# Attention with 49 agents and two split MLPs: inputs laid out transposed by the host, 25 chunks of 500 in place of 26 of 480

## The reference

```python
def sm(a, b):
    s = scale * (a @ b.transpose(0, 2, 1))
    s = s - s.max(-1, keepdims=True)
    e = np.exp(s)
    return e / (e.sum(-1, keepdims=True) + 1e-09)
agent_v = sm(agents, k) @ v            # 49 x 128, softmax over 12480 keys
x = sm(q, agents) @ agent_v            # 12480 x 128, softmax over 49 agents
h = x @ w_in                           # d_ff 2048
g = np.where(h >= 1, h, np.where(h <= -1, 0.0, (h + 1) ** 2 / 4.0))
x = g @ w_out
r = np.maximum(x @ w_in2, 0.0)
out = (s * (r * r) + b) @ w_out2
```

## Time and profile before

| what | value |
|---|---|
| median of 3 runs | 1188.39 us (1187.94 to 1191.43) |
| profiled execution, first to last instruction | 1189.1 us |
| PE busy | 1165.3 us, 98% |
| DVE, ACT, POOL busy | 954.6, 953.0, 841.0 us (80%, 80%, 71%) |
| start, to the first loop matmul (L573) | 106.6 us |
| DMA | 30.44 MB, nearly all of the reading in the first 100 us |

### The profile page before, as it was taken

The page is one execution under the profiler, slowest core; times in us unless marked ns, Lnnn a source line. Parts: engine busy times, 40 slices in busy tenths (PEclk is TensorE's granted clock), DMA queues, the critical chain, the costliest instruction groups (busy, mean ns, idle before and its releaser), DMA issues.

```text
span 1189.1 us, 20297 instructions
## 1 busy us (share of the span) xinstructions
PE 1165.3 (98%) x5668; PEld 1003.0 (84%) x5668; DVE 954.6 (80%) x1573; ACT 953.0 (80%) x1856; POOL 841.0 (71%) x1264
## 2 busy tenths in 40 slices
PE   9988899999999999999999999999999999999998
PEld 8986588888888888888888888888888888888886
DVE  2365888888888888888888888878888888888876
ACT  2225888888888888888888888888888888888886
POOL 2231088788778877887888788778877887887860
PEclk9999999999999999999999999999999999999999
DMA  7653000000000000000000000000000000000000
GB/s 187 193 141 95 1 1 18 1 17 18 17 0 17 17 17 0 17 17 1 17 17 17 1 17 17 17 1 17 17 0 17 17 17 0 18 9 9 1 9 17
DMA packets 12282, 30.44 MB, mean 26 GB/s; under 512 B 1529, under 2 KB 1578, under 8 KB 11962
## 3 DMA queue, kind: packets, MB, share of 16 engines
q1 hardware_dynamic: 12218, 29.78, 9.5%
HBM read 23.39 MB, written 6.39 MB: 25 GB/s over the span
## 4 chain that ended last, share of the span: by engine, by line
PE 87%; ACT 5%; issue 3%; DVE 3%; DMA 1%; ACTq 0%; SPq 0%; DVEq 0%
PE ps_h L592 7%; PE ps_h L593 7%; PE ps_h L594 7%; PE ps_o L634 7%; PE ps_y L554 7%; PE ps_o L635 7%; PE ps_o L636 7%; PE ps_y L556 7%; PE ps_h L573 7%; PE ps_y L555 7%; PE ps_h L574 7%; PE ps_h L455 2%; PE ps_h L443 2%; PE ps_job L455 2%; ACT sb_g_hi L732 1%
## 5 line engine op out<-in xcount | busy, mean ns | idle before, releaser
L1057 POOL TENSOR_TENSOR sb_g_lo<-sb_square,sb_g_hi 128x480 fp32r<-128x480 f32 x396 | 487.1, 1230 | 33.0
L917 DVE SCALAR_TENSOR_TENSOR ps_h<-sb_square,ps_h 128x480 f32<-128x480 f32 x416 | 274.6, 660 | 107.0 <-ACT sb_square L712 105.4
L732 ACT ACTIVATE sb_g_hi<-ps_h 128x480 fp32r<-128x480 f32 x416 | 238.4, 573 | 122.9 <-DVE ps_h L917 111.6
L900 DVE SCALAR_TENSOR_TENSOR sb_g_lo<-ps_h,sb_g_hi 128x480 fp32r<-128x480 f32 x416 | 273.0, 656 | 33.6 <-ACT sb_g_hi L732 24.0
L906 DVE TENSOR_SCALAR sb_below<-ps_h 128x480 f32<-128x480 f32 x400 | 262.0, 655 | 12.8 <-PE ps_h L574 10.2
L737 ACT ACTIVATE sb_relu<-ps_h 128x480 f32<-128x480 f32 x416 | 238.1, 572 | 21.4 <-PE ps_h L594 13.6
L712 ACT ACTIVATE sb_square<-sb_below 128x480 f32<-128x480 f32 x416 | 250.3, 602 | 0.9 <-DVE sb_below L906 0.4
L746 ACT ACTIVATE sb_square<-sb_relu 128x480 f32<-128x480 f32 x416 | 249.9, 601 | 0.6
L1055 POOL TENSOR_SCALAR sb_g_hi<-sb_square 128x480 fp32r<-128x480 f32 x396 | 232.4, 587 | 0.0
L1054 POOL TENSOR_TENSOR sb_gate<-sb_ones 1x1 f32<-1x1 f32 x396 | 73.8, 186 | 187.6 <-ACT sb_square L746 180.8
L554 PE MATMUL ps_y<-sb_g_hi,sb_w_out_hi 128*128 128x480 f32 x416 | 167.2, 402 | 2.4 <-DVE sb_g_lo L900 1.5
(11 more groups left out here) (114 smaller groups left out, 1484.6 us busy)
## 6 DMA issues: line engine op xcount, KB each, us to landing
sb_kv_ring<-in_k SPq DMA_DIRECT2D x13, 480.0 KB, 5.3
sb_q_ring<-in_q SPq DMA_DIRECT2D x26, 240.0 KB, 3.0
sb_kv_ring<-in_v SPq DMA_DIRECT2D x13, 480.0 KB, 5.6
out<-sb_out_ring SPq DMA_DIRECT2D x26, 240.0 KB, 2.4
sb_w_stage<-in_moe_w_in SPq DMA_DIRECT2D x1, 1024.0 KB, 7.2
sb_w_in<-in_moe_w_in SPq DMA_DIRECT2D x1, 1024.0 KB, 10.0
sb_w_stage<-in_moe_w_out SPq DMA_DIRECT2D x2, 0.5 KB, 11.6
sb_agents<-in_agents SPq DMA_DIRECT2D x1, 24.5 KB
```

The source lines that it names most:

```text
L732: nc.scalar.activation(g1_hi[:, place % SPLIT_RING], h1_ps[place % H1_BANKS][:, 0:W], ACT.Relu).then_inc(g1_hi_ready, 1)
L900: nc.vector.scalar_tensor_tensor(g1_lo[:, place % SPLIT_RING], h1_ps[place % H1_BANKS][:, 0:W], 0.0, as_f32(g1_hi[:, place % SPLIT_RING]), ...
L917: nc.vector.scalar_tensor_tensor(h, square1[:, place % WORK_RING], 1.0, h, ALU.min, ALU.add).then_inc(g1_summed, 1)
L1057: nc.gpsimd.tensor_tensor(g2_lo[:, place % SPLIT_RING], square, as_f32(hi), ALU.subtract).then_inc(g2_split, 1)
```

## The change

The host hands over `q` and `k` transposed (128 x tokens; `q` padded to 12500), `v` and the output weights already arranged by tile, `agents` transposed, `s` and `b` as two columns, and turns the output back itself. On the chip:

- `turn_k`, the copies to `k_t`, `turn_q`, the copy to `q_t`, the transposes of the output and their copy, and the transpose of the agents are gone.
- Keys come in 12 blocks of 8 tiles of 128 and one block of 2 tiles of 96; all of `k` has room at once, so nothing holds its loads back. The loads of `v` reuse the room of `k`.
- `weigh_v` has the values as the stationary operand (128 columns) and the exponentials moving (49 columns), and so gives `agent_v` transposed. The denominators come from `sum_exp`, one matmul with ones per block.
- A chunk is 500 tokens (4 sub-tiles of 126, overlapping), 25 chunks.
- The bias from `b` and `w_out2` comes from 16 small matmuls in iteration 0 (`sum_w_out2`) instead of a reduction on DVE; all parts of `m` are rounded by ACT and split by DVE, instead of ACT copies and POOL; `w_out1` is loaded and split in four parts; the guard of the query softmax is a 50th column.

```diff
-CHUNKS_PER_LOAD = 2
-KV_RING = 4
+W = 500
+TOK = 126
+SUB_AT = [0, TOK, 2 * TOK, W - TOK]
+KV_TILES = 8
...
+            def score_k(n):
+                keys = k_last[:] if n == KV_BLOCKS else kv_ring[:, n]
+                rows = block_rows(n)
+                pe.wait_ge(k_loaded[n], 16)
+                at_least(pe, a_scores_kept, n - SCORE_BANKS + 1)
+                for t in range(block_tiles(n)):
+                    mm = pe.matmul(score_banks[n % SCORE_BANKS][0:rows, t * n_agents:(t + 1) * n_agents],
+                                   keys[:, t * rows:(t + 1) * rows], agents_t[:], start=True, stop=True)
+                mm.then_inc(a_scored, 1)
...
-                    mm = pe.matmul(y_ps[0:n_agents, 0:C], a_exp[:, odd, t], kv_ring[:, slot, t * C:(t + 1) * C],
...
+            def sum_exp(n):
+                rows = block_rows(n)
+                pe.wait_ge(a_block_sum, n + 1)
+                pe.matmul(o_ps[:, 0:n_agents], ones[0:rows, :], a_block[0:rows, n % 2], start=(n == 0),
+                          stop=(n == KV_BLOCKS), skip_group_check=True).then_inc(a_sum_spread, 1)
...
+                    mm = pe.matmul(y_ps[:, 0:n_agents], values, a_scores[0:rows, n * KV_TILES + t],
...
-                    if j == J_TURN_Q and chunk(i, phase, 1)[2]:
-                        turn_q(i + 1, (phase + 1) % IO_RING, turns + (phase + 1) // IO_RING)
...
-                        for t in range(SUBS_PER_CHUNK):
-                            mm = pe.transpose(job_ps[0:TOK, t * C:(t + 1) * C], out_t[:, t * TOK:(t + 1) * TOK], ident[:])
-                        mm.then_inc(out_turned, 1)
...
+                    if first(i) and j >= J_BIAS:
+                        sum_w_out2(j)
...
+            def shift_block(n):
+                rows = block_rows(n)
+                nc.vector.tensor_tensor(block_scores(n), block_scores(n),
+                                        h2_ps[1][0:rows, 0:n_agents].rearrange("p (t a) -> p t a", t=1).to_broadcast([rows, block_tiles(n), n_agents]),
+                                        ALU.subtract).then_inc(a_shifted, 1)
...
+                    if first(i) and KEPT + j < len(m_parts):
+                        split_m(KEPT + j)
```

More of the change, by code:

```diff
@@ L49, with build_program @@
 IO_RING = 3
[L51 removed]
 J_SCORES = 3
[L53 removed]
 J_TURN_P = 12
[L56 to L57 removed]
+J_BIAS = 8
+W = 500
+TOK = 126
+SUBS = 4
+SUB_AT = [0, TOK, 2 * TOK, W - TOK]
+KV_TILES = 8
+LAST_TILES = 2
+LAST_TOK = 96
+SCORE_BANKS = 4
+W_PARTS = 4
 LOW = 64
[L62 to L63 removed]
+def build_program(nc, q, k, v, v_last, agents, w_in1, w_out1, w_in2, w_out2, s_b, out):
+    C, n_queries = q.shape
+    n_tokens = k.shape[1]
     n_agents = agents.shape[1]
@@ L525, in _, with keep_awake @@
-            pe.transpose(h2_ps[0][:, 0:n_agents], agent_v[:], ident[0:n_agents, 0:n_agents]).then_inc(agent_v_turned, 1)
+            def keep_awake(turns):
+                for _ in range(turns):
+                    pe.transpose(y_ps[:, 0:128], ident[:], ident[:])
+            def score_k(n):
[6 more added lines that the diff above has]
+                                   keys[:, t * rows:(t + 1) * rows], agents_t[:], start=True, stop=True)
+                mm.then_inc(a_scored, 1)
@@ L528, in _ @@
+            keep_awake(6)
+            for n in range(BLOCKS):
+                sum_exp(n)
+                if n == KV_BLOCKS:
+                    pe.wait_ge(consts_ready, 6)
+                    turn_probs(0)
+                weigh_v(n)
             pe.wait_ge(agent_v_t_ready, 2)
-            pe.wait_ge(bias_ready, 1)
             pe.wait_ge(w_in1_loaded, 16)
@@ L539, in _, with sum_w_out2 @@
                 make_m(n)
+            def sum_w_out2(j):
+                if j == J_BIAS:
+                    pe.wait_ge(w_out2_loaded, 16)
+                    pe.wait_ge(scales_loaded, 16)
+                    pe.wait_ge(m_split, 3)
+                for f in range((j - J_BIAS) * 2, (j - J_BIAS) * 2 + 2):
+                    mm = pe.matmul(o_ps[:, 0:1], w_stage[0][:, f * 128:(f + 1) * 128], s_b_cols[:, 1:2],
+                                   start=(f == 0), stop=(f == TILES - 1))
+                if j == TILES - 1:
+                    mm.then_inc(bias_summed, 1)
             def multiply_g1(i, phase, j, lag):
@@ L690, in keep_probs @@
+            for n in range(BLOCKS):
+                keep_scores(n)
+            act.wait_ge(consts_ready, 6)
+            exp_q(0)
+            for n in range(BLOCKS):
+                exp_block(n)
             def keep_probs(c, slot):
@@ L1068, with turned, by_tile @@
     from concourse.bass_utils import run_bass_kernel_spmd
+    def turned(x, columns):
+        rows, C = x.shape
+        a = np.zeros((C, columns), dtype=x.dtype)
+        a[:, 0:rows] = x.T
+        return a
+    def by_tile(x, tok):
+        rows, C = x.shape
+        return np.ascontiguousarray(x.reshape(rows // tok, tok, C).transpose(1, 0, 2).reshape(tok, rows // tok * C))
+    q, k, v, agents = (inputs[name][0] for name in ("q", "k", "v", "agents"))
+    n_tokens = q.shape[0]
+    full = n_tokens - LAST_TILES * LAST_TOK
+    laid = {
+        "q": turned(q, -(-n_tokens // W) * W),
+        "k": turned(k, n_tokens),
+        "v": by_tile(v[:full], 128),
+        "v_last": by_tile(v[full:], LAST_TOK),
+        "agents": turned(agents, agents.shape[0]),
+        "moe_w_in": np.ascontiguousarray(inputs["moe_w_in"]),
+        "moe_w_out": by_tile(inputs["moe_w_out"], 128),
+        "moe2_w_in": np.ascontiguousarray(inputs["moe2_w_in"]),
+        "moe2_w_out": by_tile(inputs["moe2_w_out"], 128),
+        "moe2_s_b": np.ascontiguousarray(np.broadcast_to(np.concatenate([inputs["moe2_s"], inputs["moe2_b"]]), (128, 2))),
+    }
     nc = bacc.Bacc("TRN2", target_bir_lowering=False, num_devices=1)
```

518 lines of the change are left out of this document (178 added, 340 removed).

## The result

| | median | runs |
|---|---|---|
| before | 1189.62 us | 4, 1187.94 to 1191.43 |
| changed | 1169.65 us | 4, 1167.16 to 1172.12 |

The ratio is 0.984, 95% interval 0.9818 to 0.9862: 20.0 us faster. The forecast was 1163, the time 6.6 us above it, within the range of 1137 to 1176. The likeliest case came true in its kind (the low clock in the value stage, the loop bound by PE), but the time says little for that: several terms were off and partly cancelled.

A forecast was written before the change was run, and what follows sets the result against it. PE was taken to bound the kernel, except ACT in iteration 0. From the profiled 1189.1 us, -2.0 - 21.7 - 1.4 + 0.3 - 5.9 + 5.1 = -25.6 gave 1163.5, stated as 1163; range 1137 to 1176.

The forecast's parts named there:

- The likeliest case: Whole kernel: the forecast itself, PE bounding the loop and a low clock in the value stage; 1154 to 1171 us, 60%.
- Turns in the loop, -21.7: Loop from iteration 1 on: without query and output transposes, PE's extras fall from 51.1 to 29.4 us, -21.7 us.
- Matmul count and width, -2.0: Loop: 4576 matmuls of 480 columns at 0.219 us become 4400 of 500 at 0.2273, -2.0 us.
- Leaves 0.2 for the turns of the loop.: Loop: 40.65 us of a measured 40.85 us chunk explained; the other 0.2 us taken as looping cost of every chunk.
- Key stage, 0.41 a tile: Key scores: lower clock level, 98 tiles at 0.41 us, 40.2 us in all, from 5.9 to 46.1 us.
- Value stage, 45.5 us: Weighing of values: lower clock level, 98 tiles at 0.41 us and 13 `sum_exp` at 0.41, 45.5 us.
- Iteration 0, +5.1: First iteration: low clock +2.4, DVE's splits of `m` ahead of sums +1.5, `sum_w_out2` +1.0, ACT +0.2; +5.1 us.
- End, -1.4 + 0.3: Last output without transposes and copy, -1.4 us; first and last items grow with the width, +0.3 us.
- 1, the clock in the value stage: Clock rises before or in the value stage, which takes 23 us instead of 45.5; kernel 1141 us, 20%.
- 2: Loop: the matmul's period depends on weight loads, not on width; kernel 1126 us, 8%.
- 3: PE stays at the lower clock level beyond iteration 0; one and a half such chunks give 1214 us, 4%.
- 4, the start gives less: Start: narrow matmuls dearer than 0.41 us, or weights late for iteration 0; kernel 1180 us, 8%.

The follow-up runs named there:

- e5: Changed kernel with eight transposes of the identity put back in every iteration, behind the same waits, results unread: 1188.4 us, +18.75.
- e4: Changed kernel with all iterations written out as straight code, without a loop or branch: 1161.33 us, -8.3.
- e2: Changed kernel with ACT rounding the next part of `m` at an item's end and DVE splitting it behind the sum: 1166.06 us, -3.6.
- e6: Changed kernel with exponentials stationary (49 columns) and values moving (128), `agent_v` divided and turned after: 1146.82 us, -22.8.
- e1: Changed kernel with 20 `keep_awake` transposes instead of 6 ahead of the values: 1166.09 us, -3.6.
- e3: Changed kernel with 26 chunks of 480 (sub-tiles of 120) instead of 25 of 500: 1174.41 us, +4.8.
- e9: Changed kernel with 30 chunks of 416 (sub-tiles of 104) instead of 25 of 500: 1184.98 us in a single run.
- e8: Changed kernel with eight identity transposes behind each block of key scores and 20 instead of 13 ahead of the first: 1161.47 us, -8.2.

## Why the prediction was right, and where it was not

**Span and launch.** The forecast had 1163.5 us for the profiled execution; its span is 1167.8, 4.3 more. Another 1.8 us is the step from the span to the launch's time (1169.62 for that run), which the earlier trace rows don't show and the forecast left out: it went 0.7 down instead. 4.3 + 1.8 + 0.5 (that 0.7, less rounding) are the 6.6.

**Turns in the loop, -21.7.** Right: 0.88 us a chunk measured by e5 against 0.86. In the whole kernel e5 finds 18.75, since at the branches part of a transpose fills time that PE would wait anyway.

**Matmul count and width, -2.0.** The mechanism is right, and the spacing to 0.8 ns: 226.5 against 227.3. An ordinary chunk follows from it: 176 x 0.2265 + 1.28 is 41.14, and 41.19 was measured. But over 4400 matmuls 0.8 ns are 3.5 us: by the measured spacings the term is 996.6 - 1001.2 = -4.6.

**"Leaves 0.2 for the turns of the loop."** This step failed. The forecast spread the cost of a branch evenly over the chunks and carried it over. The chain of the kernel before would have told them apart:

```profile
263.72 0.78 PE ps_job L417 x8
345.70 0.78 PE ps_job L417 x8
386.32 0.78 PE ps_job L417 x8
```

An ordinary chunk there is 40.62 us, two with a branch between are 81.98, so a branch cost 0.74. In the changed kernel it costs 1.48 us, and e4 gets 8.2 us back for six of them, where 21 x 0.2 are 4.2. With less work on PE per iteration, more of the stall of ACT behind the branch comes through: 0.9 with e5's transposes, 1.48 without. (In the kernel before, with 0.74, ACT's stall was itself shorter, 1.5 to 1.8 us in the chain; why was not tested.) The full chunks take 873.9 instead of 871.5, +2.4: each ordinary one 0.3 less than the 41.5 forecast, and each of six branches 1.48 more.

**Key stage, 0.41 a tile.** Right in kind, but a tile at the low level costs 0.427. The forecast took 0.193 us an instruction from a whole load's 3.08 / 16, which holds one short first step. Inside such a load the steps are longer, as the timeline of the kernel before shows:

```profile
43.65 2.00 PE L455 MATMUL ps_job<-sb_agents_t,sb_k_t 128*120 128x49 f32 x9
45.45 1.83 PE L443 MATMUL ps_h<-sb_ident,sb_kv_ring 120*128 120x120 f32 x8
```

Nine instructions in 1.80 us are 0.200 each; in proportion to the stationary columns that is 0.213 for 128, 0.427 a tile. All at the low level the stage would have taken 41.8 us (e2, e6), not 40.2. It took 38.9, since the first 3 us ran at the high level in this execution, and it ended at 43.9 instead of 46.1. The forecast had no such stretch, so that part is luck. The transfers ran at some 410 GB/s (10 to 30 us), not at the 245 taken; they were covered either way.

**Value stage, 45.5 us.** The level was right: the twelve transposes did not raise the clock. e1 adds that twenty, which do, would not have kept it up: with 49 moving columns it fell back within some 6 us. The forecast took a value tile for the same as a key tile, which is right, but both are 0.427, not 0.41. With the 0.8 of the probabilities the stage took 48.1 instead of 46.3. The dearer tiles and the luck in the key stage cancel: 100.37 against 100.7. In e2's profile, without that luck, the same point comes at 103.36.

**Iteration 0, +5.1.** This is the step that failed most, by 3.1: it took 38.4 us instead of 30.2, +8.2. "I estimate +1.5" for DVE's order was one split of delay. In the trace each item closes a loop through both engines, PE waits 5.33 us in one piece, and the clock falls once more; e2 takes 6.4 us off by the order alone, over iterations 0 and 1. The forecast did price the low level (+2.4), but once and from the start of the iteration, not again after the wait.

**End, -1.4 + 0.3.** The last output is right at -1.4. Iteration 1 and the end together took 155.1 us, 0.9 less than the 156.0 that the forecast left for them. So the 4.3 us of the span are -0.3 (start), +3.1 (iteration 0), +2.4 (full chunks) and -0.9.

**The rivals.** 1, the clock in the value stage: not as the change was made, but e6 shows what it was worth, 22.8 us, close to the 22 worked out for it. 2 is refuted by e3 and e9. 3 did not happen: the second low stretch ended at 118 us, inside iteration 0. 4, the start gives less: its mechanism did happen, narrow matmuls at 0.427 instead of 0.41, some 3 us for 196 tiles, but the high stretch in the key stage hid it, and the start gave -6.2.

**The clock and the rule of the Trainium skill.** The prediction cited "TensorE: Matmul & The Clock Gate", section "Part 4: PE-mode transpose", by which transposes don't count as PE-busy for the clock, and said that the rows spoke against it. The runs do so clearly: in e8, with 8 transposes a block, PE runs 187 instructions in 20 us of the key stage instead of 95; in e1 the granted clock reads 1.00 behind 20 of them, and a block takes 1.95 us instead of 3.61. The measurements decide.

## What to carry to other kernels

Whether PE is busy does not tell its clock: before pricing a stage, look at whether the durations of a known shape there are those of the high or the low level, and try the wide operand as the moving one; turning a small matmul round saved a transpose here and cost 22.8 us. A gap of a few microseconds in front of PE, as in the first iteration of a pipeline, should be priced with the slow matmuls that may follow it (after 5.33 us here they did, after 1.98 in one profile of two). When work is taken off the full engine, ask what lay beside it: here a stall at each branch of the loop, which had been partly covered, came out.

## What the runs showed of the hardware that was not expected

- PE without an idle moment was at the lower level (1.2 GHz) for all but some 3 of 39 us in the key stage (in e2 and e6 for all 42) and for all 48 of the value stage with 128 stationary and 49 moving float32 columns, and fell back to it from the higher level in e1 while working on nothing else. With 49 stationary and 128 moving columns it rose by itself (e6).
- Useless transposes between the narrow matmuls made the stage faster: 2.61 us in place of 3.41 a block, with half as many instructions again (e8).
- At the low level a tile of 128 stationary and 49 moving float32 columns costs 0.427 us, both where each tile has its own columns of a bank (key stage of e2) and where all tiles accumulate in one place (value stage). At the high level it is 1.72 / 8 = 0.215 in e8's key stage.
- fp32r matmuls with a weight load each are 189.7, 218.8 and 226.5 ns apart at N = 416, 480 and 500 columns: N / 2.4 ns and 16 to 19 ns more.
- Behind a branch of the loop ACT does nothing for 1.9 to 2.1 us, with no wait that the profile shows; written out (e4) the loop has no such stall.
- Behind the same first transposes the clock is high in some executions and not in others, which is worth 3 us of the total (41.81 against 38.88 us in the key stage); the printed granted clock can be 1.00 over instructions that run at the low level.
